# Separate steps for shifts and local exponentials, scores ahead of values from unit 10 on, and other places for the weights' high parts

## The chip, the cores and the metric

One core of a Trainium2 chip runs the whole program. The metric is the device time of one execution in microseconds, as the median of several runs. The engines are TensorE (PE, with its weight loads as PEld), VectorE (DVE), ScalarE (ACT), GpSimd (POOL) and SyncE (SP), which issues the DMAs. Each engine works through its own list of instructions in order and waits on semaphores.

## What is computed

Attention of two kinds over 4 batches of 8 heads, 576 tokens, head size 64, and behind it two layers over the 2304 tokens:

```python
def _attn_ref(q, k, v):                       # 4, 8, 576, 64
    q_d, k_d, v_d = (a.reshape(B, H, S // 4, 4, D).mean(axis=3) for a in (q, k, v))
    out_up = np.repeat(sm_attn(q_d, k_d, v_d), 4, axis=2)      # pooled
    mask = np.abs(pos[:, None] - pos[None, :]) < 4             # local
    scores = np.where(mask, scale * q @ k.T, -1e9)
    ...
    attn = softmax(scores)
    return out_up + attn @ v
def _moe_ref(x, w1, w2, w3, w_out):           # 512 -> 768 -> 512
    return np.maximum(np.maximum(x @ w1, x @ w2), x @ w3) @ w_out
def _moe2_ref(x, w_in, w_out):                # 512 -> 2048 -> 512
    h = x @ w_in
    return np.maximum(0.01 * h, h) @ w_out
```

## The kernel before, in words

**Attention.** Two heads at a time make a pair, four pairs a batch. The pairs of the first batch are cut into a front and a back part; all others are whole. This makes 20 units (`UNITS`): 0 to 3 front, 4 to 7 back, 8 to 19 whole. A unit goes through these items:

- D (DVE, `group_sums`): sums of four keys and four queries, for the pooled scores.
- S (PE, `scores`): pooled scores into banks 2 and 3 of `att_ps`, then local scores into banks 0 and 1.
- H (DVE, `shifts`): first the maximum over the pooled scores (line 1742), which releases ACT; then for the local scores the mask's addition (line 1746), the maximum (line 1753) and the subtraction (line 1757).
- E (ACT, `exps`): the bias from the pooled maximum, the pooled exponentials (line 1410), which empty banks 2 and 3, then a wait for the subtraction on DVE, and the local exponential (line 1416).
- N and NG (DVE and ACT, `normalise`): sums, reciprocals and scaling of the probabilities.
- T (PE, `transposes`; ACT, `transposed`): pooled probabilities transposed into bank 3 (line 1113 or 1117), local ones into banks 1 and 2 (line 1124). ACT evacuates them.
- V (PE, `values`; ACT, `up`): the pooled values, which ACT copies into `upT`, and the local values. A (DVE, `combine`) adds both into `x_raw`.

**First product.** The tokens are cut into four chunks, 288, 288, 480 and 480 wide, and the rest follows in another form. A chunk is 22 groups: for each of 6 blocks three groups for w1, w2 and w3, then four groups of w_out. M(g) is group g; M0 to M21 belong to chunk 0, M22 to M43 to chunk 1, M44 on to chunk 2. Each product is made in three passes of high and low parts (lines 1199 to 1201): operand = high + low, where ACT writes the high part and DVE or POOL the low part by a subtraction. A group of w1 is evacuated by ACT (`half_max`, line 1546), one of w2 or w3 by DVE (lines 1841 and 1845). The result's high part is ACT's (line 1472) and its low part DVE's (line 1827).

**Banks.** Four `mlp_ps` banks serve the groups of the first product. From group 22 to 77 the value banks av0 and av1 of whole units come out of the same four, in turn (`_turn`, `MIXED`). Each job waits in `begin` until the job before it in its bank has been evacuated.

**Weights.** W(c, s) is one step of weight chunk c. Chunks 0 to 5 (w1, w2, w3) have two steps, chunks 6 to 11 (w_out) one. ACT writes the high part (line 1558), then POOL the low part, in four pieces for a step of chunks 0 to 5 and two for the others (line 956). PE waits for POOL's pieces of chunk f at the group of w1 of block f of chunk 0, which is M(3f) (line 1213), and for all of them at M18 (line 1219).

**Order.** `first_phase` writes one list of items by hand: `put(at, ...)` gives each a place, counted in groups of the first product, and the list is sorted by it, in order of `put` where places are equal. Each engine takes its own items out of the one sorted list. `plan` holds for each unit u the places of N, T, of the scores of unit u + 2 and of V. `shifted_at` puts H and E of some units behind their scores. For units from 12 on whose scores and values have the same place, `scores_first` puts S(u + 2) ahead of V(u), and the order on DVE is H(u + 2), A(u). A changed order also changes which job is ahead of which in a bank.

Of the kernel before, what the change touches and what calls it, by code (L numbers as in the profile page):

```python
# [35 lines left out]
TQ = 64  # L36
# [111 lines left out]
def first_phase():  # L148
# [5 lines left out]
    def put(at, *names):  # L154
# [6 lines left out]

    put(0, ("LQ", 0), ("LQ", 1), ("LR", 0), ("LQ", 2), ("LV", 0), ("LR", 1), ("LQ", 3), ("LV", 1), ("WL", 0),
# [31 lines left out]
    for u, (n_at, t_at, s_at, v_at) in plan.items():  # L194
# [8 lines left out]
        scores_first = s_at == v_at and u >= 12  # L203
        if not scores_first and s_at == v_at:
            put(v_at, ("V", u), ("A", u))
        if s_at is not None:
            put(s_at - {7: 1.95, 9: 2.1}.get(u, 1.5), ("D", u + 2))
            put(s_at, ("S", u + 2))
            if scores_first:
                put(v_at, ("V", u))  # L210
            h_at = shifted_at.get(u + 2, s_at)
            put(h_at, ("H", u + 2))
            put(h_at + (0.02 if scores_first else 0.1 if u + 2 in shifted_at else 0.5), ("E", u + 2))
# [177 lines left out]
def build(nc, kq_parts, kq_whole, v_parts, v_whole, v_rest, v_band, w123, w_out, v_in, v_out, out, y_dram, u_dram):  # L391
    with ExitStack() as ctx:
# [1003 lines left out]
        def _(act):  # L1396
            def exps(u):
                part = UNITS[u][1]
                tiles, n = PART_GROUPS[part], 2 * len(PART_SLOTS[part][0])
# [13 lines left out]
                last.then_inc(exp_done, 1)  # L1413
# [290 lines left out]
        def _(dve):  # L1704
# [22 lines left out]
            def shifts(u):  # L1727
# [4 lines left out]
                if u == PAIRS:  # L1732
                    dve.wait_ge(mask_ready, 3)
# [359 lines left out]
```

## Time and profile before

| | us |
|---|---|
| median of 3 runs | 761.29 |
| lowest and highest | 760.94, 761.37 |
| profiled execution | 762.59 |
| its span, first to last instruction | 760.8 |
| PE busy | 751.5 |
| DVE busy | 446.4 |
| ACT busy | 307.4 |
| POOL busy | 167.9 |

The profile is of one execution, by the hardware profiler. Busy time is time in which an instruction of the engine was under way; for a line of several equal instructions the duration is from the first's start to the last's end. Matmuls overlap: the start of the next comes well ahead of the modelled end of the one before, so a stall of PE is read from the step between starts. In brackets stands how long the engine had been idle and what released it; this is inferred from semaphores, and of several it is the last.

### The profile page before, as it was taken

To read this page: it belongs to the slowest core of one execution; us is meant where nothing else is said; L and a number is where in the kernel's file an instruction comes from. 1 tells how busy PE (TensorE), PEld (TensorE's weight loads), DVE (VectorE), ACT (ScalarE), POOL (GpSimd) and SP (SyncE) were. 2 spreads that over 40 slices of the span, in tenths; PEclk is the share of its full clock that TensorE was granted. 3 is DMA by queue.
4 is the path that set the end of the run, shared out by engine and by line. 5 is a ranking of instruction groups with operands and counts; after the bars stand their busy time and mean duration, and the time that the engine had idled before them with its cause. 6 is when DMAs were issued, how large, how long until landed. Compare 5 with 4: busy or idle time off the path is not lost.

```text
span 760.8 us, 13983 instructions
## 1 busy us (share of the span) xinstructions
PE 751.5 (99%) x5580; PEld 681.2 (90%) x5580; DVE 446.4 (59%) x769; ACT 307.4 (40%) x733; POOL 167.9 (22%) x209
## 2 busy tenths in 40 slices
PE   8999999999999999999999999999999999999998
PEld 7889999888888889999999888898898989889896
DVE  6877788767644734667665566573334465344433
ACT  4675645535424323343534544442222243223222
POOL 3985121211111433431344433200000000000000
PEclk9999999999999999999999999999999999999999
DMA  8643433323121024213469545446322345223402
GB/s 287 199 178 104 149 114 109 98 81 123 43 65 35 17 79 124 63 32 112 145 249 356 194 153 188 158 175 247 132 97 97 106 163 202 98 96 114 164 14 83
DMA packets 42192, 99.73 MB, mean 131 GB/s; under 512 B 6768, under 2 KB 27248, under 8 KB 39056
## 3 DMA queue, kind: packets, MB, share of 16 engines
q1 hardware_dynamic: 42128, 98.84, 37.1%
q8 instruction: 44, 0.72, 0.4%
q14 instruction: 20, 0.16, 0.1%
HBM read 74.71 MB, written 24.12 MB: 130 GB/s over the span
## 4 chain that ended last, share of the span: by engine, by line
PE 91%; DVE 4%; ACT 1%; issue 1%; DMA 1%; POOL 0%; SPq 0%; DVEq 0%; ACTq 0%
PE mlp_ps L1199 10%; PE mlp_ps L1201 9%; PE mlp_ps L1200 9%; PE mlp_ps L1351 8%; PE mlp_ps L1353 8%; PE mlp_ps L1352 8%; PE att_ps L1372 6%; PE att_ps L1374 6%; PE att_ps L1373 6%; PE mlp_ps L1374 3%; PE mlp_ps L1373 3%; PE mlp_ps L1372 3%; PE att_ps L1271 2%; PE att_ps L1273 2%; PE att_ps L1272 2%
## 5 line engine op out<-in xcount | busy, mean ns | idle before, releaser
L1199 PE MATMUL mlp_ps<-x_hi,wa_lo 128*128 128x288 f32 (+1 forms) x288 | 101.1, 351 | 0.6 <-ACT half_max L1546 0.5
L1201 PE MATMUL mlp_ps<-x_hi,wa_hi 128*128 128x288 f32 (+1 forms) x288 | 97.4, 338 | 0.0
L1200 PE MATMUL mlp_ps<-x_lo,wa_hi 128*128 128x288 f32 (+1 forms) x288 | 97.1, 337 | 0.0
L1644 ACT ACTIVATE h_last_a<-wa_raw 128x384 fp32r<-128x384 f32 x72 | 37.7, 524 | 104.8 <-DVE wa_raw L1980 104.2
L1978 DVE TENSOR_TENSOR wa_raw<-mlp_ps,h_raw 128x384 f32<-128x384 f32 x24 | 13.4, 557 | 80.1 <-PE mlp_ps L1353 51.8
L1199 PEld LDWEIGHTS mlp_ps<-x_hi,wa_lo 128*128 128x128 f32 x288 | 54.1, 188 | 6.4 <-ACT half_max L1546 0.8
L1201 PEld LDWEIGHTS mlp_ps<-x_hi,wa_hi 128*128 128x128 f32 x288 | 54.1, 188 | 4.6
L1200 PEld LDWEIGHTS mlp_ps<-x_lo,wa_hi 128*128 128x128 f32 x288 | 54.2, 188 | 4.1
L1992 DVE TENSOR_TENSOR h_last_b<-wa_raw,h_last_a 128x384 fp32r<-128x384 f32 x72 | 43.8, 611 | 23.4 <-ACT h_last_a L1644 21.1
L1374 PE MATMUL att_ps<-wa_hi,h_last_a 128*128 128x512 f32 x132 | 52.2, 396 | 0.0
L1373 PE MATMUL att_ps<-wa_lo,h_last_a 128*128 128x512 f32 x132 | 52.1, 395 | 0.0
L935 POOL TENSOR_TENSOR v_rows<-v_rows 128x512 f32<-128x512 f32 x12 | 15.8, 1319 | 138.3 <-DMA v_rows<-in_v_rest 138.3
L1623 ACT ACTIVATE half_max<-mlp_ps 128x384 f32<-128x384 f32 x48 | 23.5, 490 | 28.1 <-PE mlp_ps L1353 28.1
L1199 PE MATMUL mlp_ps<-h_hi,wo_lo 128*128 128x288 f32 (+1 forms) x96 | 33.0, 344 | 0.0
L1351 PE MATMUL mlp_ps<-early_hi,u_odd 128*128 128x384 f32 x96 | 32.8, 342 | 0.0
L1351 PE MATMUL mlp_ps<-early_hi,u_even 128*128 128x384 f32 x96 | 32.8, 341 | 0.0
L1353 PE MATMUL mlp_ps<-early_hi,u_odd 128*128 128x384 f32 x96 | 32.7, 340 | 0.0
L1353 PE MATMUL mlp_ps<-early_hi,u_even 128*128 128x384 f32 x96 | 32.7, 340 | 0.0
L1201 PE MATMUL mlp_ps<-h_hi,wo_hi 128*128 128x288 f32 (+1 forms) x96 | 32.5, 339 | 0.0
L1200 PE MATMUL mlp_ps<-h_lo,wo_hi 128*128 128x288 f32 (+1 forms) x96 | 32.4, 338 | 0.0
L1352 PE MATMUL mlp_ps<-early_lo,u_odd 128*128 128x384 f32 x96 | 32.4, 338 | 0.0
L1352 PE MATMUL mlp_ps<-early_lo,u_even 128*128 128x384 f32 x96 | 32.4, 337 | 0.0
(226 smaller groups left out, 2067.9 us busy)
## 6 DMA issues: line engine op xcount, KB each, us to landing
u_even<-u_scratch SPq DMA_DIRECT2D x8, 1792.0 KB, 7.5
u_odd<-u_scratch SPq DMA_DIRECT2D x8, 1792.0 KB, 7.3
kq_in<-in_kq_whole SPq DMA_DIRECT2D x12, 608.0 KB, 4.6
u_scratch<-u_even SPq DMA_DIRECT2D x4, 1792.0 KB, 9.0
u_scratch<-u_odd SPq DMA_DIRECT2D x4, 1792.0 KB, 9.2
wa_raw<-in_w SPq DMA_DIRECT2D x6, 768.0 KB, 6.6
v_win<-in_v_band SPq DMA_DIRECT2D x12, 384.0 KB, 3.3
ws_raw<-in_w SPq DMA_DIRECT2D x18, 256.0 KB, 3.4
```

The costliest lines, as they stand in the source:

```text
L1199: nc.tensor.matmul(ps, wlo, xhi, start=(n == 0), stop=False)
L1200: nc.tensor.matmul(ps, whi, xlo, start=False, stop=False)
L1201: last = nc.tensor.matmul(ps, whi, xhi, start=False, stop=(n == len(pairs) - 1))
L1351: nc.tensor.matmul(ps, wlo[:, k], xhi[:, k], start=(first and k == 0), stop=False, skip_group_check=True)
L1352: nc.tensor.matmul(ps, whi[:, k], xlo[:, k], start=False, stop=False, skip_group_check=True)
L1353: last = nc.tensor.matmul(ps, whi[:, k], xhi[:, k], start=False, stop=(k == KT - 1), skip_group_check=True)
L1372: nc.tensor.matmul(ps, glo, hi, start=(f == 0), stop=False)
L1373: nc.tensor.matmul(ps, ghi, lo, start=False, stop=False)
L1374: last = nc.tensor.matmul(ps, ghi, hi, start=False, stop=(f == NF2 - 1))
L1623: nc.scalar.activation(p_copy[i], l1_bank(quad, i == 2), ACT.Copy).then_inc(copied, 1)
L1644: nc.scalar.activation(g_tile(0, quad, part), g_raw[part], ACT.Copy).then_inc(g_hi_ready, 1)
L1992: nc.vector.tensor_tensor(g_tile(1, quad, part), g_raw[part], g_tile(0, quad, part).bitcast(F32), ALU.subtract).then_inc(g_split, 1)
```

## The change

The diff:

- H is split: `maxima` keeps the wait for the pooled scores and their maximum under the name H, `shifts` has the local part under the name K. E is split in the same way: `exps` keeps bias and pooled exponentials, `local_exps` (item L) has the local exponential.
- For units 0 to 9 and 13, H and K stay together. E and L stay together there too, except that L13 has a later place with nothing of ACT between. L10 moves behind M24 and V8 on ACT, L11 behind M28 and V9.
- Where S(u + 2) and V(u) have one place and no `shifted_at` applies, which is u = 10 and 12 to 17, the order in the list is S(u + 2), V(u), H(u + 2), E(u + 2), A(u), K(u + 2), L(u + 2). On PE this puts S12 ahead of V10; on DVE it is now H, A, K, where it was A, H, K for unit 12 and H, K, A for units 14 to 19.
- Unit 13 goes by `shifted_at`; on PE S13 now comes ahead of V11, on DVE its order stays.
- On ACT the high parts move: W(3,1) from behind M3 to behind M6; W(4,0) from ahead of T4 to behind E6; W(4,1) from behind M6 to behind V4; W(5,0) from ahead of V4 to behind M9; W(5,1) from behind M9 to behind M10; W(10,0) from behind NG7 to ahead of E8; W(11,0) from behind V6 to behind NG7. POOL's and SP's lists stay as they were.
- The same instructions are issued as before.

```diff
--- before.py
+++ after.py
@@ -159,25 +159,26 @@
 
 
 
+
     put(0, ("LQ", 0), ("LQ", 1), ("LR", 0), ("LQ", 2), ("LV", 0), ("LR", 1), ("LQ", 3), ("LV", 1), ("WL", 0),
-        ("Z", 8), ("D", 0), ("D", 1), ("S", 0), ("H", 0), ("Z", 5), ("E", 0), ("D", 2), ("G", 0), ("S", 1), ("H", 1), ("Z", 6), ("E", 1),
-        ("LR", 2), ("G", 1), ("N", 0), ("NG", 0), ("S", 2), ("H", 2), ("Z", 2), ("T", 0), ("Z", 3), ("E", 2), ("D", 3), ("LR", 3), ("WL", 1),
-        ("V", 0), ("A", 0), ("W", 0, 0), ("W", 0, 1), ("LV", 2), ("XH", 0, 0), ("N", 1), ("NG", 1), ("XL", 0, 0), ("S", 3), ("H", 3), ("Z", 2), ("G", 2), ("T", 1),
-        ("Z", 3), ("E", 3), ("G", 3), ("W", 1, 0), ("N", 2), ("NG", 2), ("V", 1), ("A", 1), ("Z", 8), ("LV", 3), ("WL", 2), ("T", 2), ("XH", 0, 1), ("N", 3), ("NG", 3),
+        ("Z", 8), ("D", 0), ("D", 1), ("S", 0), ("H", 0), ("K", 0), ("Z", 5), ("E", 0), ("L", 0), ("D", 2), ("G", 0), ("S", 1), ("H", 1), ("K", 1), ("Z", 6), ("E", 1), ("L", 1),
+        ("LR", 2), ("G", 1), ("N", 0), ("NG", 0), ("S", 2), ("H", 2), ("K", 2), ("Z", 2), ("T", 0), ("Z", 3), ("E", 2), ("L", 2), ("D", 3), ("LR", 3), ("WL", 1),
+        ("V", 0), ("A", 0), ("W", 0, 0), ("W", 0, 1), ("LV", 2), ("XH", 0, 0), ("N", 1), ("NG", 1), ("XL", 0, 0), ("S", 3), ("H", 3), ("K", 3), ("Z", 2), ("G", 2), ("T", 1),
+        ("Z", 3), ("E", 3), ("L", 3), ("G", 3), ("W", 1, 0), ("N", 2), ("NG", 2), ("V", 1), ("A", 1), ("Z", 8), ("LV", 3), ("WL", 2), ("T", 2), ("XH", 0, 1), ("N", 3), ("NG", 3),
         ("W", 1, 1), ("XL", 0, 1), ("Mk", 0, 0, 1), ("Mk", 1, 0, 1), ("Mk", 2, 0, 1), ("V", 2), ("A", 2), ("T", 3), ("D", 4),
         ("Mk", 0, 1, 2), ("Mk", 1, 1, 2), ("Mk", 2, 1, 2), ("LV", 4), ("WL", 3), ("X", 0, 2),
         ("V", 3), ("A", 3), ("D", 5), ("LV", 5), ("WL", 4), ("WL", 5), ("Mk", 0, 2, 3), ("Mk", 1, 2, 3), ("Mk", 2, 2, 3),
-        ("X", 0, 3), ("W", 2, 0), ("S", 4), ("H", 4), ("E", 4), ("Mk", 3, 0, 3))
+        ("X", 0, 3), ("W", 2, 0), ("S", 4), ("H", 4), ("K", 4), ("E", 4), ("L", 4), ("Mk", 3, 0, 3))
     for i in range(NF1):
         put(4, ("WL", NF1 + i))
     put(0.5, ("W", 2, 1))
-    for c, at in ((3, 2.95), (4, 5.4), (5, 8.4)):
+    for c, at, then in ((3, 2.95, 6.02), (4, 7.6, 8.7), (5, 9.2, 10.1)):
         put(at, ("W", c, 0))
-        put(at + 1, ("W", c, 1))
-    for c, at in ((6, 10.3), (7, 11.3), (8, 12.7), (9, 13.7), (10, 14.7), (11, 15.7)):
+        put(then, ("W", c, 1))
+    for c, at in ((6, 10.3), (7, 11.3), (8, 12.7), (9, 13.2), (10, 14.1), (11, 14.75)):
         put(at, ("W", c, 0))
     put(0, ("LQ", 4))
-    put(2.2, ("S", 5), ("H", 5), ("E", 5))
+    put(2.2, ("S", 5), ("H", 5), ("K", 5), ("E", 5), ("L", 5))
     put(1.5, ("LQ", 5))
     put(13.0, ("C", 0))
 
@@ -200,23 +201,23 @@
         put(n_at, ("N", u))
         put(n_at + (scaled.get(u, 1.1) if part == WHOLE else 0), ("NG", u))
         put(t_at, ("T", u))
-        scores_first = s_at == v_at and u >= 12
-        if not scores_first and s_at == v_at:
-            put(v_at, ("V", u), ("A", u))
+        merged = s_at == v_at
         if s_at is not None:
             put(s_at - {7: 1.95, 9: 2.1}.get(u, 1.5), ("D", u + 2))
             put(s_at, ("S", u + 2))
-            if scores_first:
-                put(v_at, ("V", u))
-            h_at = shifted_at.get(u + 2, s_at)
-            put(h_at, ("H", u + 2))
-            put(h_at + (0.02 if scores_first else 0.1 if u + 2 in shifted_at else 0.5), ("E", u + 2))
             q = UNITS[u + 2][0]
             if u + 2 >= WHOLE0 and q + 2 < NPAIR:
                 put(s_at + 0.4, ("LQ", q + 2))
-        if scores_first:
-            put(v_at + 0.03, ("A", u))
-        elif s_at != v_at:
+        if merged and u + 2 not in shifted_at:
+
+            put(v_at, ("V", u), ("H", u + 2), ("E", u + 2), ("A", u), ("K", u + 2))
+            put(v_at + 0.02, ("L", u + 2))
+        else:
+            if s_at is not None:
+                h_at = shifted_at.get(u + 2, s_at)
+                put(h_at, ("H", u + 2), ("K", u + 2))
+                put(h_at + (0.1 if u + 2 in shifted_at else 0.5), ("E", u + 2))
+                put(h_at + {10: 0.9, 11: 1.0}.get(u + 2, 0.5), ("L", u + 2))
             put(v_at, ("V", u), ("A", u))
         if u + 2 < NU:
             put(v_at, ("LV", u + 2))
@@ -1396,7 +1397,7 @@
         def _(act):
             def exps(u):
                 part = UNITS[u][1]
-                tiles, n = PART_GROUPS[part], 2 * len(PART_SLOTS[part][0])
+                tiles = PART_GROUPS[part]
                 nq, ng = tiles[0][1], len(tiles)
                 act.wait_ge(max_ready, u + 1)
                 nc.scalar.activation(bias_g[:nq, u % 2, 0:2 * ng], row_max[:nq, SLOTS:SLOTS + 2 * ng], ACT.Copy,
@@ -1411,6 +1412,9 @@
                                                 bias=bias_g[:nq, u % 2, i:i + 1], scale=SCALE / FACTOR ** 2,
                                                 accum_out=row_sum[:nq, u % 2, SLOTS + n_i:SLOTS + n_i + 1])
                 last.then_inc(exp_done, 1)
+
+            def local_exps(u):
+                n = 2 * len(PART_SLOTS[UNITS[u][1]][0])
                 act.wait_ge(shifted, u + 1)
                 local = prob_l[:, u % 2, 0:n, :]
                 nc.scalar.activation(local, local, ACT.Exp, scale=SCALE).then_inc(exp_done, 1)
@@ -1591,6 +1595,8 @@
             for item in FIRST:
                 if item[0] == "E":
                     exps(item[1])
+                elif item[0] == "L":
+                    local_exps(item[1])
                 elif item[0] == "NG":
                     normalise(item[1])
                 elif item[0] == "T":
@@ -1724,22 +1730,25 @@
 
                     dve.wait_ge(att_done, JOB[f"lt{len(LT[UNITS[u - 2][1]]) - 1}", u - 2] + 1)
 
+            def maxima(u):
+                tiles = PART_GROUPS[UNITS[u][1]]
+                nq, ng = tiles[0][1], len(tiles)
+                dve.wait_ge(att_done, JOB["sg1", u] + 1)
+                src = att_ps[:nq, 2:4, 0:ng * SD].rearrange("p h (n i) -> p h n i", i=SD)
+                max_g = row_max[:nq, SLOTS:SLOTS + 2 * ng]
+                if u:
+
+                    dve.wait_ge(bias_ready, u)
+                nc.vector.tensor_reduce(max_g.rearrange("p (h n) -> p h n", h=2), src, AX.X, ALU.max).then_inc(max_ready, 1)
+
             def shifts(u):
                 part = UNITS[u][1]
-                tiles, (m0, m1) = PART_GROUPS[part], PART_MASK[part]
-                nq, ng, ns = tiles[0][1], len(tiles), len(PART_SLOTS[part][0])
+                (m0, m1), ns = PART_MASK[part], len(PART_SLOTS[part][0])
                 local = prob_l[:, u % 2, 0:2 * ns, :]
                 if u == PAIRS:
                     dve.wait_ge(mask_ready, 3)
                 scores = att_ps[:, 0:2, 0:ns * TQ].rearrange("p h (s w) -> p h s w", w=TQ)
                 by_head = local.rearrange("p (h s) w -> p h s w", h=2)
-                dve.wait_ge(att_done, JOB["sg1", u] + 1)
-                src = att_ps[:nq, 2:4, 0:ng * SD].rearrange("p h (n i) -> p h n i", i=SD)
-                max_g = row_max[:nq, SLOTS:SLOTS + 2 * ng]
-                if u:
-
-                    dve.wait_ge(bias_ready, u)
-                nc.vector.tensor_reduce(max_g.rearrange("p (h n) -> p h n", h=2), src, AX.X, ALU.max).then_inc(max_ready, 1)
                 dve.wait_ge(att_done, JOB["sl1", u] + 1)
                 if part != FRONT:
                     place_free(u)
@@ -1942,6 +1951,8 @@
                 if item[0] == "D":
                     group_sums(item[1])
                 elif item[0] == "H":
+                    maxima(item[1])
+                elif item[0] == "K":
                     shifts(item[1])
                 elif item[0] == "N":
                     normalise(item[1])
```

## Rows read from the trace of the kernel before

**Rows 1.** The page of before: busy time, share of the span and instructions of each engine.

```profile
PE 751.5 (99%) x5580; PEld 681.2 (90%) x5580; DVE 446.4 (59%) x769; ACT 307.4 (40%) x733; POOL 167.9 (22%) x209
```

**Rows 2.** Table by stage: window, its us, PE, PEld, DVE, ACT, POOL busy, PEclk (granted clock), DMA share, GB/s.

```profile
120.00:160.00 40.00, 40.00 (x540) 36.50 (x540) 32.10 (x56) 20.53 (x66) 4.07 (x4) 1.00 0.35 112
```

**Rows 3.** Timeline around S6, all engines. Columns: start us, duration us, engine, line, operation.

```profile
42.11 0.63 DVE L1827 TENSOR_TENSOR h_lo<-h_raw,h_hi 128x288 fp32r<-128x288 f32 x1 [1.39 <-ACT h_hi L1472]
42.27 1.57 ACT L1558 ACTIVATE wa_hi<-wa_raw 128x768 fp32r<-128x768 f32 x2
43.52 0.38 DVE L1714 TENSOR_REDUCE kq_sum<-x_raw 128x57 f32<-128x228 f32 x1
44.20 0.21 PEld L1088 LDWEIGHTS att_ps<-kq_sum 64*57 64x57 f32 x4 [1.01 <-DVE kq_sum L1714]
44.23 0.46 PE L1088 MATMUL att_ps<-kq_sum 64*57 64x144 f32 x4 [0.80 <-ACT probT_g L1440]
```

**Rows 4.** Timeline around M18, POOL and PE.

```profile
66.91 3.03 POOL L956 TENSOR_TENSOR wo_lo<-wo_raw,wo_hi 128x256 fp32r<-128x256 f32 x4 [3.68 <-ACT wo_hi L1558]
69.72 0.29 PE L1201 MATMUL mlp_ps<-x_hi,wa_hi 128*128 128x288 f32 x1
70.04 0.37 PE L1199 MATMUL mlp_ps<-h_hi,wo_lo 128*128 128x288 f32 x1
```

**Rows 5.** Timeline around T10 and M30: ACT, PE's weight load, DVE.

```profile
102.22 0.55 PE L1113 MATMUL att_ps<-ident,prob_g 72*128 72x72 f32 x6
102.44 0.74 ACT L1416 ACTIVATE prob_l<-prob_l 128x640 f32<-128x640 f32 x1 [0.67 <-DVE prob_l L1757]
103.41 0.39 ACT L1546 ACTIVATE half_max<-mlp_ps 128x288 f32<-128x288 f32 x1
103.70 0.28 ACT L1455 ACTIVATE upT<-mlp_ps 128x144 f32<-128x144 f32 x1
103.86 0.19 PEld L1199 LDWEIGHTS mlp_ps<-x_hi,wa_lo 128*128 128x128 f32 x1 [0.78 <-ACT half_max L1546]
104.02 0.31 DVE L1788 TENSOR_TENSOR upT<-mlp_ps,upT 128x144 f32<-128x144 f32 x1 [1.61 <-ACT upT L1455]
```

**Rows 6.** Timeline, 105 to 109.5 us: POOL's add, DVE's low part and group sums.

```profile
105.50 1.29 POOL L935 TENSOR_TENSOR v_rows<-v_rows 128x512 f32<-128x512 f32 x1 [7.26 <-DMA v_rows<-in_v_rest]
105.58 1.53 DVE L1827 TENSOR_TENSOR h_lo<-h_raw,h_hi 128x288 fp32r<-128x288 f32 x1
108.00 1.41 DVE L1714 TENSOR_REDUCE kq_sum<-kq_in 128x304 f32<-128x1216 f32 x1
```

**Rows 7.** Timeline, 108 to 117 us: V10, S12, H12, E12, T11.

```profile
108.86 0.47 PE L1152 MATMUL mlp_ps<-probT_g,v_mean 64*64 64x144 f32 x8
109.84 0.70 PE L1079 MATMUL att_ps<-kq_sum 64*64 64x144 f32 x16
113.76 0.75 DVE L1742 TENSOR_REDUCE row_max<-att_ps 72x4 f32<-72x576 f32 x1
115.56 0.30 PE L1199 MATMUL mlp_ps<-x_hi,wa_lo 128*128 128x288 f32 x1
...
115.83 0.29 PE L1201 MATMUL mlp_ps<-x_hi,wa_hi 128*128 128x288 f32 x1
116.13 0.20 ACT L1410 ACTIVATION_READ_ACCUMULATOR prob_g<-att_ps,bias_g 72x1 f32 x1
116.48 0.57 PE L1113 MATMUL att_ps<-ident,prob_g 72*128 72x72 f32 x6 [0.36 <-ACT prob_g L1410]
```

**Rows 8.** Timeline, 119 to 121 us: D13 on DVE and V11 on PE.

```profile
119.68 1.40 DVE L1714 TENSOR_REDUCE kq_sum<-kq_in 128x304 f32<-128x1216 f32 x1
120.72 0.47 PE L1152 MATMUL mlp_ps<-probT_g,v_mean 64*64 64x144 f32 x8
```

**Rows 9.** Timeline, 140 to 148 us: V12's pooled output on ACT, M46 on DVE.

```profile
141.93 0.29 ACT L1455 ACTIVATE upT<-mlp_ps 128x144 f32<-128x144 f32 x1 [1.63 <-PE mlp_ps L1187]
147.44 0.66 DVE L1845 TENSOR_TENSOR h_raw<-mlp_ps,h_raw 128x480 f32<-128x480 f32 x1 [1.68 <-PE mlp_ps L1201]
```

More of the change, by code:

```diff
@@ L1725, in place_free @@
                     dve.wait_ge(att_done, JOB[f"lt{len(LT[UNITS[u - 2][1]]) - 1}", u - 2] + 1)
-            def shifts(u):
-                part = UNITS[u][1]
-                tiles, (m0, m1) = PART_GROUPS[part], PART_MASK[part]
-                nq, ng, ns = tiles[0][1], len(tiles), len(PART_SLOTS[part][0])
-                local = prob_l[:, u % 2, 0:2 * ns, :]
-                if u == PAIRS:
-                    dve.wait_ge(mask_ready, 3)
-                scores = att_ps[:, 0:2, 0:ns * TQ].rearrange("p h (s w) -> p h s w", w=TQ)
-                by_head = local.rearrange("p (h s) w -> p h s w", h=2)
+            def maxima(u):
+                tiles = PART_GROUPS[UNITS[u][1]]
+                nq, ng = tiles[0][1], len(tiles)
                 dve.wait_ge(att_done, JOB["sg1", u] + 1)
@@ L1742, in shifts @@
                 nc.vector.tensor_reduce(max_g.rearrange("p (h n) -> p h n", h=2), src, AX.X, ALU.max).then_inc(max_ready, 1)
+            def shifts(u):
+                part = UNITS[u][1]
+                (m0, m1), ns = PART_MASK[part], len(PART_SLOTS[part][0])
+                local = prob_l[:, u % 2, 0:2 * ns, :]
+                if u == PAIRS:
+                    dve.wait_ge(mask_ready, 3)
+                scores = att_ps[:, 0:2, 0:ns * TQ].rearrange("p h (s w) -> p h s w", w=TQ)
+                by_head = local.rearrange("p (h s) w -> p h s w", h=2)
                 dve.wait_ge(att_done, JOB["sl1", u] + 1)
```

## Prediction, written before the changed kernel was run

> Items are called as in the plan: M9 is group 9 of the first product, S12, V12 and T12 are scores, values and transposes of unit 12, H, K, E, L, A, N, D its maxima, shifts, the two exponential steps, combination, normalisation and group sums, and W(c, s) is step s of weight chunk c. The unit in S, H, K, E, L and D is two ahead of the one in V and A beside it.
>
> **What bounds the kernel now.** The page comes first: PE is busy for 751.5 of 760.8 us [rows 1]. The table by stage comes next: from 120 us on PE is busy in every slice at a granted clock of 1.00, here its upper level of 2.4 GHz, while DVE and ACT have air [rows 2]. So nothing on DVE or ACT can give time back there, only take some. What a change of order can win is PE's stalls before 120 us. I looked for them in PE's timeline, as steps between two starts that are longer than usual; a bracket alone understates them, since a matmul's modelled end overlaps the next start. The usual step of 288-wide matmuls is 0.13 us (115.56 to 115.83 are two) [rows 7]. Behind 40 us four places stand out:
> - S6, 44.23: PE sat for 0.80, put down to ACT's evacuation of T4. The weight load beside it names DVE's kq_sum (D6) instead [rows 3].
> - M18, 70.04: 0.32 after the last matmul, so 0.19 too late. POOL's last low part ended at 66.91 + 3.03 = 69.94, and M18 waits for it at line 1219 [rows 4].
> - M30, 103.86: the weight load idled for 0.78 until ACT's half_max of M28, whose bank it takes [rows 5].
> - T11, 116.48: 0.65 after the last matmul, so 0.52 too late. Its bank held S12's pooled scores, and E12, which frees it, ended at 116.13 + 0.20 = 116.33 [rows 7].
>
> These four hold 2.29 us with S6 at its 0.80, and that is nearly all that is to be had.
>
> **Weights' high parts.** Nothing is added: the same 12 high steps run on ACT, seven at other places. POOL's own order does not change, but its low parts wait for the high ones. SP's order does not change at all.
> At S6: W(3,1) and W(4,0), two steps in 1.57 us from 42.27, stood ahead of T4's evacuation; now both come behind it, which can start near 42.3 and is over by 43. What is late next is D6: 43.52 + 0.38 = 43.90. The operations ahead of it on DVE begin with the low part at 42.11, which waited for an h_hi that stands on ACT ahead of both moved steps, so D6 does not move. From the evacuation (43.74 + 0.34 = 44.08, an ACT row of the same view) to the load at 44.20 passed 0.12; the same behind D6 puts it at 44.02. Gain **0.18**, not 0.80 [rows 3]. The ends are 0 and 0.80; I take 0.18 as D6 has a row of its own.
> Its price is on POOL: W(3,1) now starts behind M6's half_max, near 44.3, and ends near 45.1. Its four low pieces take at most 0.76 each (3.03/4, for pieces a third wider) [rows 4], so they are done by 48.1. M9, which waits for them at line 1213, comes behind S6, M7, M8 (24 steps of 0.13) and V4; with 0.46 for the pooled part of S6 [rows 3] alone that is 47.6, and S6's local part and V4 add an estimated 0.8: 48.4. Covered by 0.3, by an upper bound for POOL; without that cover it costs what is lacking.
> At M18: POOL idled 3.68 before 66.91, for W(10,0). This now stands ahead of E8, and W(11,0) takes its old place, so only two of the four pieces are left from 66.9: 66.91 + 1.52 = 68.4, which is 1.5 before PE needs them. What POOL lost earlier is less than the 3.68. Gain **0.19** [rows 4]; PE is now 0.37 early.
>
> **L10 and L11 later.** On ACT the local exponential of unit 11 stood ahead of M28's h_hi and half_max, and waited 0.67 for K11. ACT was therefore free at 102.44 - 0.67 = 101.77. Now h_hi (0.33), half_max (0.29) and upT of V9 (0.28) follow E11 at once: half_max is over at 101.77 + 0.72 = 102.5, 0.6 before M30's undisturbed place at 103.08. With everything 0.37 earlier that distance stays. Gain **0.78** [rows 5]. L10's move does the same in front of M25, where PE did not wait: nothing. L11 itself slips behind upT, and is needed only by N11: nothing.
> It also changes DVE. A9 had waited 1.61 for upT; now upT ends at 101.77 + 0.90 = 102.67 instead of 103.98, less 0.37. So A9 starts near 102.35 instead of 104.02: **DVE is 1.67 earlier**.
>
> **H12 ahead of A10, S12 ahead of V10 (and S13 ahead of V11).** V and S together take PE equally long either way. H12 now stands ahead of A10 and no longer waits for V10. A combination takes 1.56 (A9, 104.02 to the next operation at 105.58) [rows 5, 6]. At T11: H12 in its place of before less that 1.56 and less DVE's 1.67 ends near 111.3; E12 came 1.8 behind it (114.51 to 116.33), so it is over by 113.2. PE wants T11 at 116.48 - 0.52 - 0.37 - 0.78 = 114.8. Gain **0.52** [rows 7].
> What is late next is the group sum: S12 now stands where V10 stood, one V (108.86 to 109.84, 0.98) sooner. PE wants it at 109.84 - 0.98 - 1.15 = 107.7. D12 ended at 109.41, 1.67 earlier 107.74. But the low part at 105.58 took 1.53, under POOL's 105.50 to 106.79; now it starts at 103.9, ahead of that. D12 is then held only by M30's end (102.7, twelve steps and a tail of 0.3: 104.6), the h_raw behind it and its own 1.41, and ends near 106.7. Covered by 1.0 [rows 6, 7].
> S13 likewise: PE wants it at V11's place, 120.72 - 1.67 = 119.05. D13 ended at 119.68 + 1.40 = 121.08 and has DVE's 1.67 and A10's unchanged length behind it, plus at least the 1.07 just said: 118.3. Covered by 0.7 [rows 8]. If neither relief came, it would cost up to 0.4 here.
>
> What the row says of sharing: the same kind of operation, 128x288 from two SBUF tensors, took 1.53 beside POOL and 0.63 at 42.11 [rows 3, 6]. The Trainium skill, "SBUF — State Buffer", section on the two separate sides, says that a DVE operation with two SBUF inputs and a GpSimd one that reads SBUF shut each other out for a whole instruction. Row and rule agree, and the rule speaks against the change in one thing: a reorder can put another such operation under POOL's.
>
> **K behind A from unit 14 on.** H14, A12, K14 replaces H14, K14, A12. DVE then idles until V12's upT, which ends at 142.22; before, K14 filled that gap. The idle time is between 0 and 1.9 (ACT's wait of 1.63 and the 0.29). Behind it DVE had waited 1.68 for M46 at 147.44, and no bank that PE wants frees sooner by it [rows 9]. So it costs 0, six times. L14's wait on ACT is longer too, with the same cover.
>
> **Sum.** 0.18 + 0.19 + 0.78 + 0.52 = 1.67 us. The profiled execution took 762.59 with a span of 760.8, 1.8 outside; its span would be 759.1. The median of the runs is 761.29, 1.3 below that execution; I carry the difference over: 761.29 - 1.67 = **759.6**.
>
> **Rivals.**
> - A, S6 gives all: if D6 is not what ends the wait, the full 0.80 goes. 759.0. For it: PE's row names ACT. Against: the load's row and 43.90.
> - B, new waits for the group sums: D12 or D13 late at S12 and S13, since these stand 1.0 sooner. If DVE gains nothing but PE's 0.37, D12 ends at 109.04 and S12 waits 1.3; S13 another 0.3. Then the gains at M30 and T11 are given back: 760.9. Against: A9's 1.61 of waiting is real.
> - C, POOL's add meets another operation of DVE with two SBUF inputs, the low part ahead of D12 or D13: 1.07 late, of which 1.0 and 0.7 are covered. PE waits 0.1 to 0.5: 760.0. The skill's rule named above is this one.
> - D, slower: K behind A. If DVE's idle time is more than what M46 left, 1.68, each of six units hands PE the rest. From 0.5 each on (an idle time of 2.2) it costs 3 us or more and outweighs all: 763. Against: the upper bound is 1.9, and PE takes a bank again only groups later.
>
> **How the numbers follow.** Forecast 0.55, A 0.10, B 0.17, C 0.13, D 0.05. The range reaches from a little below A to B: 758.8 to 761.1; D and the edge of B are left out. About 0.2% (1.5 us) is what a measurement of this kernel can tell from no change; that line is at 759.8, only 0.15 above the forecast, so a quarter of the forecast's own chance and most of C count as no change. Faster 0.54, same 0.41, slower 0.05.
>
> **What would show it.** S6 starts with its wait put down to kq_sum near 44.0; M18 follows its forerunner by 0.13; M30's load has no idle time behind half_max; T11 has no wait for E12; S12 and S13 start without one for kq_sum; PE's busy time from 120 us on stays full. A wait for kq_sum at S12 or S13 over 0.3, or any at M9, or a PE gap behind 130 us, makes the prediction wrong.

## The result and the profile after

| | before | changed |
|---|---|---|
| median of 20 runs | 761.50 | 762.98 |
| lowest and highest | 760.72, 763.69 | 762.34, 765.84 |
| profiled execution | 762.59 | 763.77 |
| its span | 760.8 | 762.0 |

The ratio is 1.002, with a 95% interval of 1.0013 to 1.0028: the changed kernel is slower by 1.0 to 2.1 us. The forecast was 759.6, with a range up to 761.1.

The lines of the changed kernel are up to nine numbers further down (PE's 1113 is 1114, its 1124 is 1125, its 1199 is 1200; ACT's 1410, 1416 and 1424 are 1411, 1420 and 1428; DVE's 1714, 1757, 1769 and 1815 are 1720, 1766, 1778 and 1824). The page's busy times say little: PE 751.9, DVE 447.6, ACT 307.5 and POOL 167.9 us, all within 1.2 us of those before [rows 1].

The table by stage says more. From 120 to 160 us PE is full in both kernels [rows 2]; from 160 to 240 it is not. The columns are the window, its us, PE, PEld, DVE, ACT and POOL busy, granted clock, DMA share and GB/s. First the kernel before:

```profile
160.00:240.00 80.00, 80.00 (x856) 68.97 (x855) 47.53 (x87) 33.37 (x104) 10.15 (x10) 1.00 0.22 69
```

Then the changed one:

```profile
120.00:160.00 40.00, 40.00 (x539) 36.59 (x537) 30.48 (x53) 20.12 (x65) 4.95 (x6) 1.00 0.35 118
160.00:240.00 80.00, 78.70 (x848) 67.40 (x846) 47.61 (x86) 32.80 (x101) 10.13 (x10) 1.00 0.20 66
```

PE lacks 1.3 us there at a granted clock of 1.00, the upper level of 2.4 GHz; so it stood still and did not run slower. The view of waits, PE alone, 30 to 240 us, names who kept it. It gives the tile, the line, the releaser, us in total, times, and the longest:

```profile
PE att_ps L1114 <- ACT prob_g L1428: 1.3, 2, 1.1
PE att_ps L1125 <- DVE x_raw L1824: 0.8, 1, 0.8
PE att_ps L1089 <- DVE kq_sum L1720: 0.5, 1, 0.5
```

The first two lines are new, and the third is S6. The waits for `half_max` (M30) and for the pooled exponential (T11) are gone.

Both kernels issue the same matmuls, so the start of the n-th in one trace can be set against the start of the n-th in the other. This gives PE's delay against the kernel before, at any place. A step in it is time lost or won there:

| place | step, us |
|---|---|
| T3, 29 us | +0.69 |
| S6, 44 us | -0.32 |
| T7, 68 us | +0.77 |
| M18, 70 us | -0.19 |
| M30, 103 us | -0.86 |
| T11, 115 us | -0.51 |
| M40, 128 us | -0.15 |
| T15, 177 us | +0.42 |
| T18, 232 us | +1.30 |
| a bank near 396 us | +0.43 |

The changed execution was 0.45 ahead at 26 us and 1.14 behind at 401 us. The step at T3 belongs to the execution and not to the change (last section). The one at 396 us (a wait for ACT's `half_max`) was in five of the twelve profiles, with 0.3 to 0.4 in four and 1.0 in one; that of experiment 4 with its nearly old order is among them, and no run was made for its cause. M40's is a gain that nobody forecast, in a stretch where PE counts as fully busy in both kernels: by the trace its low part on DVE was just late before, and is 1.1 us earlier now, PE 0.9. No run tested this alone. The gain is in the traces of all runs but experiment 4, which has A10, H12 and L11 in their old order.

**What came.** S6, M18, M30 and T11, in PE's timeline:

```profile
44.19 0.34 PE L1089 MATMUL att_ps<-kq_sum 64*57 64x144 f32 x2 [0.53 <-DVE kq_sum L1720]
...
70.41 0.30 PE L1202 MATMUL mlp_ps<-x_hi,wa_hi 128*128 128x288 f32 x1
70.54 0.29 PE L1200 MATMUL mlp_ps<-h_hi,wo_lo 128*128 128x288 f32 x1
...
103.03 0.71 PE L1125 MATMUL att_ps<-ident,prob_l 128*128 128x128 f32 x5
103.50 0.38 PE L1200 MATMUL mlp_ps<-x_hi,wa_lo 128*128 128x288 f32 x1
...
115.51 0.29 PE L1202 MATMUL mlp_ps<-x_hi,wa_hi 128*128 128x288 f32 x1
115.64 0.35 PE L1114 MATMUL att_ps<-ident,prob_g 72*128 72x72 f32 x3
```

M18 follows its forerunner by 0.13 (before 0.32) [rows 4]. M30 follows T10 at once (before 0.78 of idling) [rows 5]. T11 follows by 0.13 (before 0.65) [rows 7]. S6 still waits, now for D6 and not for the evacuation [rows 3].

**T15 and T18.** ACT, then PE:

```profile
173.83 0.74 ACT L1420 ACTIVATE prob_l<-prob_l 128x640 f32<-128x640 f32 x1 [2.22 <-DVE prob_l L1766]
175.42 1.32 ACT L1428 ACTIVATE prob_g<-prob_g,row_inv 72x144 f32<-72x144 f32 x4
...
230.66 0.74 ACT L1420 ACTIVATE prob_l<-prob_l 128x640 f32<-128x640 f32 x1 [2.50 <-DVE prob_l L1766]
231.31 1.32 ACT L1428 ACTIVATE prob_g<-prob_g,row_inv 72x144 f32<-72x144 f32 x4
...
176.80 0.60 PE L1114 MATMUL att_ps<-ident,prob_g 72*128 72x72 f32 x6 [0.23 <-ACT prob_g L1428]
232.68 0.60 PE L1114 MATMUL att_ps<-ident,prob_g 72*128 72x72 f32 x6 [1.07 <-ACT prob_g L1428]
```

The same two operations ahead of T18 in the kernel before:

```profile
228.60 0.73 ACT L1416 ACTIVATE prob_l<-prob_l 128x640 f32<-128x640 f32 x1
229.22 1.33 ACT L1424 ACTIVATE prob_g<-prob_g,row_inv 72x144 f32<-72x144 f32 x4
...
231.99 0.54 PE L1113 MATMUL att_ps<-ident,prob_g 72*128 72x72 f32 x6
```

ACT's list has L19 and then NG18. L19 waits for K19, and K19 is now behind A17 on DVE. L19 therefore starts 2.06 later, NG18 ends at 232.63 instead of 230.55, and T18, which has to have it, starts at 232.68. Before, the distance from NG18's end to T18 was 1.44. K16 behind A14 does the same to L16, NG15 and T15, where the distance was 1.22 (NG15 ended at 176.20, T15 began at 177.42).

**T7.** POOL, DVE, ACT and PE in the changed kernel:

```profile
63.23 3.40 POOL L957 TENSOR_TENSOR wo_lo<-wo_raw,wo_hi 128x256 fp32r<-128x256 f32 x4
63.47 1.18 DVE L1766 TENSOR_TENSOR prob_l<-prob_l,row_max 128x640 f32<-128x640 f32 x1
65.38 0.58 DVE L1778 TENSOR_SCALAR row_sum<-row_sum 128x14 f32<-128x14 f32 x1
66.27 0.72 ACT L1428 ACTIVATE prob_g<-prob_g,row_inv 57x144 f32<-57x144 f32 x2 [0.85 <-DVE row_inv L1783]
68.05 0.20 ACT L1461 ACTIVATE upT<-att_ps 128x57 f32<-128x57 f32 x1
68.28 0.46 DVE L1824 TENSOR_TENSOR x_raw<-att_ps,upT 128x116 f32<-128x116 f32 x2 [1.36 <-ACT upT L1461]
68.70 0.41 PE L1125 MATMUL att_ps<-ident,prob_l 128*128 128x128 f32 x2 [0.85 <-DVE x_raw L1824]
```

POOL and DVE there in the kernel before:

```profile
61.80 1.42 POOL L956 TENSOR_TENSOR wo_lo<-wo_raw,wo_hi 128x256 fp32r<-128x256 f32 x2
63.55 0.83 DVE L1757 TENSOR_TENSOR prob_l<-prob_l,row_max 128x640 f32<-128x640 f32 x1
65.10 0.17 DVE L1769 TENSOR_SCALAR row_sum<-row_sum 128x14 f32<-128x14 f32 x1
```

POOL makes four low parts from 63.23 on, those of W(9) and W(10). Before, those of W(9) were done by then, and it stood idle until 66.91 [rows 4]. So W(9)'s low parts come 1.43 later than before, although its high part was put earlier, and W(10)'s come earlier. K8's subtraction on DVE takes 1.18 instead of 0.83, beside W(9)'s; N7's small TENSOR_SCALAR takes 0.58 instead of 0.17, beside W(10)'s. ACT's `upT`, behind NG7, comes at 68.05 instead of 67.36. A6 waits for that, and the second half of T7 for the bank that A6 reads.

### The profile page after: what moved, and what is told of

Read it like the earlier page. It is cut to its first block, busy times and chain, and to the rows that moved or that the text cites. A ratio compares the mean times of both kernels' runs of the same rounds, so it can differ in the third digit from the quotient of the medians.

```text
span 762.0 us, 13983 instructions
## 1 busy us (share of the span) xinstructions
PE 751.9 (99%) x5580; PEld 681.1 (89%) x5580; DVE 447.6 (59%) x769; ACT 307.5 (40%) x733; POOL 167.9 (22%) x209
## 4 chain that ended last, share of the span: by engine, by line
PE 88%; DMA 4%; DVE 3%; ACT 2%; issue 1%; SPq 1%; POOL 0%; DVEq 0%; ACTq 0%
PE mlp_ps L1200 9%; PE mlp_ps L1202 9%; PE mlp_ps L1201 9%; PE mlp_ps L1352 7%; PE mlp_ps L1354 7%; PE mlp_ps L1353 7%; PE att_ps L1373 6%; PE att_ps L1375 6%; PE att_ps L1374 6%; PE mlp_ps L1375 3%; PE mlp_ps L1374 3%; PE mlp_ps L1373 3%; PE att_ps L1272 2%; PE att_ps L1274 2%; PE att_ps L1273 2%; DMA wa_raw<-in_w 2%
```

## The experiments

Theory Q, for T15 and T18: what is lost there is the place of NG15 and NG18 behind the longer wait of L on ACT. Its rival is D of the prediction: DVE's idle time hands PE late banks. Theory P, for T7: POOL's low parts now stand beside K8 and N7 on DVE and make them longer. Its rival (R): the high parts take ACT's time ahead of NG7.

**1. K ahead of A again, for units 14 to 19** (changed kernel otherwise).

```diff
-            put(v_at, ("V", u), ("H", u + 2), ("E", u + 2), ("A", u), ("K", u + 2))
+            k_first = u >= 12
+            put(v_at, ("V", u), ("H", u + 2), *[("K", u + 2)] * k_first, ("E", u + 2), ("A", u),
+                *[("K", u + 2)] * (not k_first))
```

> The changed kernel with K ahead of A again for units 14 to 19; everything else of the change stays. Theory Q (queue): with K behind A the local exponential L waits longer on ScalarE, and the scaling of the pooled probabilities queued behind it (NG15 behind L16, NG18 behind L19) reaches T15 and T18 late; in the changed kernel's trace that is 0.4 and 1.2 us of PE. Then both waits are gone, PE from 120 us to 345 us is without one, and the time falls by 1.6 to 1.8 us against the changed kernel, to about 0.1% under the kernel before plus or minus 0.1%. Rival S (order of scores and values, banks): the late waits come from the other order of units 12 and 13 and stay: same time as the changed kernel, 1.002 of before.

Measured: 761.43 against 761.90 before, ratio 0.9997 (0.9987 to 1.0007). The waits at T15 and T18 are gone, and the 0.85 at T7 stays:

```profile
172.99 0.74 ACT L1421 ACTIVATE prob_l<-prob_l 128x640 f32<-128x640 f32 x1 [0.66 <-DVE prob_l L1767]
...
228.29 0.74 ACT L1421 ACTIVATE prob_l<-prob_l 128x640 f32<-128x640 f32 x1
228.92 1.33 ACT L1429 ACTIVATE prob_g<-prob_g,row_inv 72x144 f32<-72x144 f32 x4
...
231.69 0.54 PE L1115 MATMUL att_ps<-ident,prob_g 72*128 72x72 f32 x6
```

The order of K and A alone is worth 1.72 us by the steps at T15 and T18. The medians, which come from two series of runs, say 1.55 (762.98 - 761.43), or 1.95 with each set against its own kernel before (1.48 slower, 0.47 faster). Rival S of that text falls, for the order of units 12 and 13 was left as changed. This convicts the edit, but not yet the mechanism: Q and D both expect it.

**2. W(9), W(10) and W(11) back in their old places** (changed kernel otherwise).

```diff
-    for c, at in ((6, 10.3), (7, 11.3), (8, 12.7), (9, 13.2), (10, 14.1), (11, 14.75)):
+    for c, at in ((6, 10.3), (7, 11.3), (8, 12.7), (9, 13.7), (10, 14.7), (11, 15.7)):
```

> The changed kernel with W(9,0), W(10,0), W(11,0) at their old places. Theory P (port): W(10,0) ahead of E8 lets POOL work on low parts from 63 to 67 us, beside K8 and N7 on VectorE, which took 1.18 and 0.58 us where they took 0.83 and 0.17 before; N7, NG7, upT of V6 and A6 come 0.8 later, and T7, which takes A6's bank, waits. Then K8's subtraction is back at 0.83, T7's wait falls from 0.86 to about 0.2, M18 gets its 0.2 back, net gain 0.4 to 0.6 us: 1.0013 of before. Rival A (ScalarE's queue): it is the high part standing ahead of V6's upT. That place is taken in both kernels (by W(11,0) or W(10,0)), so T7's wait would stay at 0.8.

Measured: 763.28, ratio 1.002 (1.0012 to 1.0029). The expected drop is not in the median, which stands 0.3 above the changed kernel's, from another series of runs. In the trace the wait at T7 is 0.44 instead of 0.85, and M18's 0.18 are back. So the trace gives some 0.2 net, which medians of such spread cannot show. K8 still takes 1.19, where the text expected 0.83; N7's TENSOR_SCALAR is at its old 0.17. P is half supported, and half of the wait was left to explain.

**3. Both edits.**

> Both edits of the two runs beside it. If Q and P hold and add: PE keeps the gains at S6 (0.3), M30 (0.8) and T11 (0.5) and has none of the three new waits: 1.4 to 1.7 us under the kernel before, 0.998 of it. If the gains at M30 and T11 are given back elsewhere: 1.000.

Measured: 760.95, ratio 0.9989 (0.9981 to 0.9998). PE waits 0.48 at T7 and 0.53 at S6, not at all at T15 and T18; it is 2.03 ahead of the kernel before from 129 us on and keeps that to the end, of which 0.66 were there at 26 us. The gains of the other edits last once K's loss is away.

**4. The kernel before, with only K behind A.** The weights' places, L10, L11 and the order of S and V are those of before.

```diff
         merged = s_at == v_at
+            if u in (10, 11):
+                put(v_at, ("V", u), ("A", u))
             put(s_at, ("S", u + 2))
-        if merged and u + 2 not in shifted_at:
+        if merged and u >= 12:
...
-                put(h_at + {10: 0.9, 11: 1.0}.get(u + 2, 0.5), ("L", u + 2))
+                put(h_at + (0.1 if u + 2 in (10, 11) else 0.5), ("L", u + 2))
```

> The kernel before with one part of the change: K behind A for units 14 to 19. Theory Q: T15 and T18 wait as in the changed kernel. T18's wait is 1.2 to 1.3. T15's is 0.4 or a little less; all else as before: 1.5 to 1.8 us slower, 1.002 of before. If the waits need the other parts too (PE running ahead after M30 and T11): no difference, 1.000.

Measured: 764.75, ratio 1.0034 (1.0022 to 1.0046), from five runs. The waits stand in PE's rows, with all of the kernel before's:

```profile
177.60 0.60 PE L1117 MATMUL att_ps<-ident,prob_g 72*128 72x72 f32 x6 [0.23 <-ACT prob_g L1431]
...
233.49 0.60 PE L1117 MATMUL att_ps<-ident,prob_g 72*128 72x72 f32 x6 [1.07 <-ACT prob_g L1431]
```

PE's steps there are 0.41 and 1.31, so the loss is the same with none of the other edits. The median says 2.85, more than these 1.7; the interval (1.7 to 3.5) just reaches them. This profile has the step of 0.4 at 396 us too; what the rest is stays open.

**5. K stays behind A, but NG15 goes ahead of V14's `upT`, and NG18 ahead of V17's.** This parts Q from D, for DVE's idle time stays as it is.

```diff
-    scaled = {9: 0.6, 10: 1.0, 12: 0.9, 13: 0.5, 14: 0.6}
+    scaled = {9: 0.6, 10: 1.0, 12: 0.9, 13: 0.5, 14: 0.6, 15: 0.75, 18: 0.85}
```

> The changed kernel, K still behind A, but on ScalarE NG15 is ahead of V14's upT and NG18 ahead of V17's upT, so neither stands behind a local exponential any more. Theory Q (only the queue on ScalarE made T15 and T18 late): both waits are gone though VectorE's order is the changed one; T15 and T18 start without a wait, 1.6 us under the changed kernel. Rival K (VectorE's own delay from A ahead of K is what PE feels, in banks or low parts): the two waits stay at 0.4 and 1.2.

Measured: 761.19, ratio 0.9992 (0.9971 to 1.0014). ACT and PE around T15 and T18:

```profile
173.35 0.74 ACT L1420 ACTIVATE prob_l<-prob_l 128x640 f32<-128x640 f32 x1 [2.37 <-DVE prob_l L1766]
175.78 0.54 PE L1114 MATMUL att_ps<-ident,prob_g 72*128 72x72 f32 x6
...
229.56 0.74 ACT L1420 ACTIVATE prob_l<-prob_l 128x640 f32<-128x640 f32 x1 [2.50 <-DVE prob_l L1766]
230.35 0.54 PE L1114 MATMUL att_ps<-ident,prob_g 72*128 72x72 f32 x6
```

L16 and L19 still wait 2.37 and 2.50 for K. Behind them now stand only an h_hi and a `half_max`, for which PE does not wait, and T15 and T18 wait no more: PE's lead over the kernel before is the same 1.64 at 150 and at 290 us. Q holds. D falls for these places: the idle time on DVE costs nothing by itself.

**6. POOL waits for N7's reciprocal before W(9)'s low parts** (changed kernel otherwise). ACT's list is untouched, so R expects the wait at T7 to stay.

```diff
                 pool.wait_ge(w_hi_done, W_HIGH[c] + step + 1)
+                if c == 9:
+                    pool.wait_ge(inv_ready, 8)
```

> The changed kernel with one wait more: POOL starts the low part of W(9,0) only when N7's reciprocal is done, near 66 us. The order on ScalarE is that of the changed kernel, so W(11,0)'s high part still stands ahead of V6's upT. Theory P (T7 waits because POOL's low parts delay K8 and N7 on VectorE): K8's subtraction takes 0.83, N7's addition 0.17, T7's wait falls from 0.86 to 0.2 or less plus what earlier parts leave; M18 comes late instead, by 0.5 to 1. Rival A (ScalarE's queue): T7's wait stays at 0.8.

Measured: one execution, 763.61 (before 761.77), so only the trace counts here. DVE at K8 and N7, and POOL behind them:

```profile
63.94 0.82 DVE L1768 TENSOR_TENSOR prob_l<-prob_l,row_max 128x640 f32<-128x640 f32 x1
65.50 0.17 DVE L1780 TENSOR_SCALAR row_sum<-row_sum 128x14 f32<-128x14 f32 x1
66.09 4.58 POOL L959 TENSOR_TENSOR wo_lo<-wo_raw,wo_hi 128x256 fp32r<-128x256 f32 x6 [2.35 <-DVE row_inv L1785]
```

Both operations are back at their lengths of before, and PE does not wait at T7. P holds and R falls. The hold costs 0.5 at M18, since six pieces now come at once, so it is no remedy.

**7. K ahead of A, and all high parts in their old places.** This was for the 0.4 to 0.5 at T7 that 2 and 3 had kept: the suspicion was that the later W(3) to W(5) make the whole of POOL's list late.

> The changed kernel with K ahead of A and all high parts of the weights at their old places. If the 0.3 of T7's wait that stayed in the run with only W(9) to W(11) back comes from the earlier high parts (POOL runs 1.3 us later there), T7's wait is 0.2 as in the kernel before; S6 has its 0.88 again, M18 its 0.19; M30 and T11 keep 0.78 and 0.52. By the trace 1.3 us under the kernel before from 130 us on: 0.9985 of it.

Measured: 761.31, ratio 0.999 (0.997 to 1.001). T7 follows as before, and K8 takes 0.83:

```profile
66.05 1.44 POOL L958 TENSOR_TENSOR wo_lo<-wo_raw,wo_hi 128x256 fp32r<-128x256 f32 x2
67.76 0.83 DVE L1767 TENSOR_TENSOR prob_l<-prob_l,row_max 128x640 f32<-128x640 f32 x1
```

POOL is done with W(9) at 67.49, before K8. (All of this profile is some 4.2 late, since it also had a wait of 3.09 at T3, for the last section.) In the run with W(9) to W(11) alone put back its two pieces ran from 62.34 to 64.36, and K8 from 62.58. So T7's wait has both halves of the moved weights as its cause: the later W(3) to W(5) delay POOL's list and bring W(9)'s low parts beside K8, and the earlier W(10) brings its own beside N7. What K8 and N7 took longer than before adds up to what T7 lost in each trace: 0.35 + 0.41 against 0.77 in the changed kernel, 0.36 against 0.33 in experiment 2, 0.55 against 0.55 and 0.31 against 0.31 in versions 8 and 9 below, and nothing of either in experiments 6 and 7.

**8 and 9. Two versions put together from this.** Both have K ahead of A, D6 earlier, so that S6 need not wait for it, and on ACT W(10) behind L8 and ahead of NG7, so that its low parts come behind N7 on DVE (POOL starts them at 64.59 in version 9, when N7's TENSOR_SCALAR has ended at 64.12); W(11) stays behind NG7. They differ in W(3), W(4) and item C. Version 9's edits besides K's:

```diff
-    for c, at, then in ((3, 2.95, 6.02), (4, 7.6, 8.7), (5, 9.2, 10.1)):
+    for c, at, then in ((3, 2.95, 3.95), (4, 6.02, 6.4), (5, 8.4, 9.4)):
-    for c, at in ((6, 10.3), (7, 11.3), (8, 12.7), (9, 13.2), (10, 14.1), (11, 14.75)):
+    for c, at in ((6, 10.3), (7, 11.3), (8, 12.7), (9, 13.2), (10, 14.35), (11, 14.75)):
-            put(s_at - {7: 1.95, 9: 2.1}.get(u, 1.5), ("D", u + 2))
+            put(s_at - {4: 3.1, 7: 1.95, 9: 2.1}.get(u, 1.5), ("D", u + 2))
```

Version 8 has W(3,1) at 6.02, W(4) at 6.4 and 7.6, and a zeroing of POOL's (item C) at 14.2 instead of 13.0.

> The version that the runs point to: K ahead of A, D6 ahead of M4 on VectorE (where it had idle time before the low part), W(3,1) and W(4,0) behind M6, W(4,1) to W(5,1) near their old places, W(10,0) behind L8, POOL's clearing behind W(9,0). S6 loses its wait altogether (0.88), T7's is 0.2 to 0.4, M18 has none (0.19), M30 and T11 as in the change (0.78, 0.52), nothing lost behind 120 us: 2.1 to 2.4 us under the kernel before, 0.997 of it. If a new wait takes the place of one of these, the sum is less by its size.

> The changed kernel with K ahead of A for units 14 to 19, D6 0.9 of a slot earlier, W(3) and W(4) at or near their old places, W(10) and W(11) between their old and new ones. If each loss has the cause that the runs before named, all of them are gone at once: no wait at T15 and T18, at most 0.2 us at T7 (0.73 in the run with W(3) later, whose low parts of W(9) reached into K8), at most 0.2 at S6, none at M18, M30 and T11. TensorE then stands 2.2 to 2.6 us ahead of the kernel before from 120 us on to the end; the ratio is 0.9965 to 0.9975. If instead W(9)'s place alone makes T7 late, 0.7 us of that stays there and the ratio is 0.998.

Measured: 8 gave 760.60, ratio 0.9972 (0.9952 to 0.9993); 9 gave 760.67, ratio 0.9974 (0.9957 to 0.9991). They are equal, and both beat the kernel before. All that is left of PE's waits from 30 to 240 us in version 9 is one line:

```profile
PE att_ps L1126 <- DVE x_raw L1825: 0.4, 1, 0.4
```

S6, M18, M30, T11, T15 and T18 are free. T7 was expected at 0.2, which is about what it has in the kernel before (0.18 more than the usual step), and kept 0.48 (0.73 in version 8). POOL's and DVE's rows name the cause again:

```profile
61.10 1.43 POOL L958 TENSOR_TENSOR wo_lo<-wo_raw,wo_hi 128x256 fp32r<-128x256 f32 x2
62.08 1.14 DVE L1767 TENSOR_TENSOR prob_l<-prob_l,row_max 128x640 f32<-128x640 f32 x1
```

K8 starts 0.45 before POOL's pair ends at 62.53. PE is 2.8 ahead of the kernel before at 129 us and 2.3 at 375 us, of which 0.7 were there at 26 us; what it gives back in between is one wait at 293 us, 0.5 more than in the kernel before, for another operation of ACT (`s_tmp`). It is in no other profile at this size, and its cause was not sought.

**10. Version 9, with POOL waiting for N3's multiplication before the low parts of W(1).** This was for the start-up.

```diff
                 pool.wait_ge(w_hi_done, W_HIGH[c] + step + 1)
+                if c == 1 and step == 0:
+                    pool.wait_ge(probs_ready, 4)
```

> As the run before it, and GpSimd waits for N3's multiplication on VectorE to end before it starts the low parts of W(1) (half a loop of them). If the start-up wait at T3 (0 or 0.7 us in most profiles, 3.25 us in one) comes of that multiplication standing beside GpSimd's low parts, no profile and no run shows it: the spread of the runs shrinks to under 1 us and nothing lies more than 1.5 us above the lowest. The price is at M3, which waits for W(1)'s low parts: up to 0.5 us. If the long multiplication has another cause, the spread stays as in the run without the wait (runs up to 4 us above the lowest) and the time is 0 to 0.5 us longer.

Measured: 760.45, ratio 0.9978 (0.9961 to 0.9995), runs from 759.90 to 763.59, against 759.98 to 763.94 without the wait. The spread did not shrink, and the profile had a start-up wait at T3. PE also lost 0.5 between 36 and 41 us, which it did not in version 9; the text had allowed up to 0.5 for the hold. The theory of that text fell; what took its place is in the last section.

## Why the prediction was wrong

**Right: the four gains.** S6 gave 0.32 (0.18 foretold), with the wait put down to `kq_sum` as foretold; M18 gave 0.19 (0.19), M30 0.86 (0.78), T11 0.51 (0.52). Their sum is 1.88, against 1.67; with M40's 0.15, which the prediction had ruled out by "nothing on DVE or ACT can give time back there", it is 2.03. The row of S6 that named ACT was rightly not taken at its word, so rival A did not happen.

**Right: the covers.** S12, S13 and M9 start without a wait. DVE was early enough for D12 and D13 because A9's wait for `upT` had gone with L11, as worked out. B and C did not happen where the prediction put them.

**Wrong: the step "K behind A from unit 14 on ... costs 0, six times".** It weighed DVE's idle time against the slack of the banks, and that part was true: experiment 5 keeps the idle time and loses nothing. What failed is its last sentence, that L14's longer wait on ACT has the same cover. That named the waiting instruction, but not what is queued behind it. For L16 this is NG15, and for L19 NG18, and each of them is ahead of a T on PE. The bound was to be had from rows like those of unit 19 above: NG18 ended 1.44 ahead of T18, and K19 had to fall behind A17 (1.5 us of work, from 226.53 to 228.06) and its wait for `upT`. L19 slipped by 2.06. PE, 0.56 early, wanted T18 at 231.99 - 0.56 = 231.4 and got it at 232.68. T15's step is smaller, 0.42, for L16 slipped by less: 1.52 against PE (0.54, and the 0.98 that PE was early), where L19 slipped by 2.62 (2.06 and 0.56). Less the distances of 1.22 and 1.44 that is 0.30 and 1.18, each 0.12 short of its step. Of the six units only these two have an NG soon behind L in ACT's list (behind L19 at once, behind L16 with an h_hi and a `half_max` between). So the cost is 1.7 us by the traces and 1.6 to 2.0 by the medians, where the sum had 0. Rival D had the sign and the edit right and the place wrong; its price by banks did not occur. That its 763 is what was measured is luck: it stands for 3 us of late banks, and no bank was late.

**Wrong: "What POOL lost earlier is less than the 3.68. Gain 0.19."** The gain was real, but the step weighed both moves of POOL's work only against its idle time and did not ask what DVE does beside the new places: K8, beside W(9)'s low parts, which came 1.43 later, and N7, beside W(10)'s, which came earlier. K8 is an operation like the one whose 1.53 stood in rows 6. Rival C named this mechanism and looked for it only at D12 and D13. The price at T7 was 0.77, four times the gain, and experiments 6 and 7 show it from both sides.

**What the sum should have been.** -2.03 for the gains, +0.77 at T7, +1.72 at T15 and T18: +0.5. The medians say +1.5 (1.0 to 2.1). The rest, 0.5 to 1.6, is not settled: it is as large as the loss at T7, and no experiment isolates it. The step of 0.4 at 396 us would fit a part, but it comes and goes between profiles of kernels that differ in nothing near it. The medians of experiments 1 and 3 fit their traces better: 1.55 to 1.95 against 1.72 for K, and 0.95 (0.2 to 1.4) against 1.4 for the sum of both edits.

## What to carry to other kernels

When an instruction gets a longer wait, read the list of *its* engine onward, for every unit it happens in, until the engine has idle time again; the slack to compare with is that of each item on the way which another engine wants, not the waiting one's. (Behind L16 an h_hi and a `half_max` came late without a loss on PE, and NG15 behind them cost 0.42.) Moving work on an engine with idle time is not free when its operations make those of another engine longer: look at what stands beside the new place, operation by operation, also for work that only slips because other work was moved. An edit with several parts whose times partly cancel is best undone one part at a time, because the version that keeps the gains (760.6 here, against 761.5 to 762.3 for the kernel before) is in neither of the two kernels.

## What the runs showed of the hardware

**DVE can lose to a row of POOL operations, not only to one.** In experiment 7, DVE then POOL:

```profile
27.12 4.72 DVE L1786 TENSOR_TENSOR prob_l<-prob_l,row_inv 128x384 f32<-128x384 f32 x1
27.55 4.74 POOL L958 TENSOR_TENSOR wa_lo<-wa_raw,wa_hi 128x192 fp32r<-128x192 f32 x8
```

In version 9 the same operation began at 27.11 beside the same POOL row (27.54), and took 0.89:

```profile
27.11 0.89 DVE L1786 TENSOR_TENSOR prob_l<-prob_l,row_inv 128x384 f32<-128x384 f32 x1
```

So with starts equal to 0.01 us DVE came ahead of POOL's row in one execution and, in the other, only in its last operation (27.12 + 4.72 = 31.84, against POOL's 32.29; the eighth began at 31.39). PE waited 3.09 at T3 for it. What decides this is open. The 0.89 is not undisturbed either: where nothing of POOL stood beside it, an operation of this shape took 0.56. Over the twelve profiles the 128x640 subtraction took 0.82 to 0.83 alone and at the median 1.19 beside POOL, N's TENSOR_SCALAR 0.17 and 0.38. A TENSOR_REDUCE of 128x640 took 0.81 in both places, and an addition of 128x480 that reads PSUM 0.66. By this the 0.63 at 42.11, which the prediction set against the 1.53 of rows 6, was disturbed too: a low part of POOL's ran from 41.82, and undisturbed the operation took 0.46. No term of the sum rests on it.

The hold of experiment 10 put POOL behind that operation, and it took 0.88 there. But it shrank no spread, so this is not what makes the runs differ in general.

**A late transfer goes with such a meeting.** Four of the twelve profiles have T3 0.3 to 0.35 late, which with the matmuls behind it makes 0.7 in three of them: the changed kernel's, and those of experiments 1, 6 and 10 (0.35 in the last). The same four, and no others, have ACT waiting for the first weights. ACT, POOL and DVE in the changed kernel:

```profile
18.23 1.58 ACT L1562 ACTIVATE wa_hi<-wa_raw 128x768 fp32r<-128x768 f32 x2 [0.62 <-DMA wa_raw<-in_w]
...
26.45 1.28 POOL L942 TENSOR_TENSOR v_rows<-v_rows 72x512 f32<-72x512 f32 x1
26.67 1.09 DVE L1778 TENSOR_SCALAR row_sum<-row_sum 128x14 f32<-128x14 f32 x1
28.84 0.49 PE L1118 MATMUL att_ps<-ident,prob_g 87*72 87x87 f32 x4 [0.23 <-ACT prob_g L1428]
```

The same three in the kernel before, whose transfer was in time:

```profile
18.10 1.57 ACT L1558 ACTIVATE wa_hi<-wa_raw 128x768 fp32r<-128x768 f32 x2
...
26.19 1.28 POOL L941 TENSOR_TENSOR v_rows<-v_rows 72x512 f32<-72x512 f32 x1
27.12 0.38 DVE L1769 TENSOR_SCALAR row_sum<-row_sum 128x14 f32<-128x14 f32 x1
```

The high parts come late against the rest, POOL's list behind them slips by some 0.7 against DVE's, and its add now begins just ahead of N3's TENSOR_SCALAR. That operation of 14 elements takes 1.09 and ends at 27.76, with POOL's add at 27.73. (In the kernel before it met the end of the same add: 0.38, to 27.50, and the add to 27.47.) The waits of the four were 0.62, 1.13, 0.65 and 1.08, and the TENSOR_SCALAR took 1.09, 1.15, 1.09 and 1.15. The Trainium skill, "SBUF — State Buffer", section on the two separate sides, says that of a GpSimd operation and a DVE one of the kinds that share a pair of ports with it, the one that starts first has the pair for its whole instruction; the end at 27.76 agrees. Experiment 7 does not: there DVE's recorded start at 27.12 lies ahead of all eight of POOL's low parts, and seven of them went first. That the transfer causes the step is read from twelve profiles that agree, not shown by an experiment on it.
